# Expert tiles of an attention, MLP and router kernel: three pairs of tiles first, weights standing and 256 rows moving

## What is computed

```python
def _attn_ref(q, k, v):            # q, k, v: 4 x 8 x 768 x 64
    for t in range(S):
        state = gamma * state + outer(k[:, :, t], v[:, :, t])
        y[:, :, t] = scale * (q[:, :, t] @ state)
def _moe_ref(x, w_in, w_out, alpha):       # x: 3072 x 512, w_in: 512 x 2048
    h = x @ w_in
    return (max(h, 0) + alpha * min(h, 0)) @ w_out
def _moe2_ref(x, expert_emb, tau, w1, w2): # 8 experts, w1: 512 x 1024, w2: 1024 x 512
    expert_idx = argmax(cosine(x, expert_emb) / tau, axis=1)
    gate_w = softmax(...)[expert_idx]
    for e in range(E):
        mask = expert_idx == e
        out[mask] = gate_w[mask, None] * (relu(x[mask] @ w1[e]) @ w2[e])
```

## Time and profile before

| | us |
|---|---|
| median of 3 runs | 961.7 |
| lowest, highest | 961.6, 962.18 |
| the profiled execution | 962.25 |
| its span, first to last instruction | 959.8 |
| TensorE busy in the span | 948.4 |
| VectorE, ScalarE, GpSimd busy | 578.9, 255.4, 242.5 |

### The profile page before, as it was taken

The page is one execution under the profiler, slowest core; times in us unless marked ns, Lnnn a source line. Parts: engine busy times, 40 slices in busy tenths (PEclk is TensorE's granted clock), DMA queues, the critical chain, the costliest instruction groups (busy, mean ns, idle before and its releaser), DMA issues.

```text
span 959.8 us, 16536 instructions
## 1 busy us (share of the span) xinstructions
PE 948.4 (99%) x5444; PEld 792.3 (83%) x5445; DVE 578.9 (60%) x1078; ACT 255.4 (27%) x404; POOL 242.5 (25%) x192
## 2 busy tenths in 40 slices
PE   8999999999999999999999999999999999999996
PEld 7888888888888888888888888888888888888885
DVE  5556579647973698469865878674332742523541
ACT  4222121112111211112111212332334543423541
POOL 4443214341433133413432223320000100000001
PEclk9999999999999999999999999999999999999998
DMA  8431296023001400140002203437331471423411
GB/s 306 158 132 56 89 393 223 1 88 132 0 0 57 162 0 0 44 153 1 1 27 74 110 22 132 154 118 267 132 133 44 145 279 44 145 102 117 139 42 54
DMA packets 27121, 102.58 MB, mean 107 GB/s; under 512 B 4383, under 2 KB 4767, under 8 KB 22448
## 3 DMA queue, kind: packets, MB, share of 16 engines
q1 hardware_dynamic: 19280, 83.01, 24.4%
q0 software_dynamic: 4336, 12.61, 3.4%
q10 hardware_dynamic: 3456, 6.32, 2.2%
HBM read 89.30 MB, written 26.30 MB: 120 GB/s over the span
## 4 chain that ended last, share of the span: by engine, by line
PE 94%; issue 3%; DMA 1%; POOL 0%; DVE 0%; SPq 0%; POOLq 0%; ACT 0%
PE bank L694 28%; PE bank L712 27%; PE bank L822 15%; PE bank L787 14%; PE bank L589 2%; PE bank L802 2%; PE bank L633 2%; PE bank L605 2%; PE bank L679 1%; PE bank L622 1%; DMA attention<-in_qk 1%; DMA expert_rows<-rows,slot_i 0%; POOL expert_rows L1553 0%; DVE en_all L908 0%; DMA rows<-expert_rows 0%
## 5 line engine op out<-in xcount | busy, mean ns | idle before, releaser
L694 PE MATMUL bank<-activations_split,weights_split 128*128 128x512 f32 x1152 | 277.9, 391 | 0.0
L712 PE MATMUL bank<-weights_split,activations_split 128*128 128x512 f32 x1152 | 276.3, 389 | 0.0
L712 PEld LDWEIGHTS bank<-weights_split,activations_split 128*128 128x128 f32 x1152 | 216.1, 188 | 45.1 <-POOL activations_split L1535 0.4
L694 PEld LDWEIGHTS bank<-activations_split,weights_split 128*128 128x128 f32 x1152 | 215.0, 188 | 45.8 <-issue 1.1
L1535 POOL TENSOR_TENSOR activations_split<-scratch,activations_split 128x512 fp32r<-128x512 f32 x84 | 116.9, 1391 | 313.1 <-ACT activations_split L1314 302.5
L1314 ACT CAST activations_split<-scratch 128x512 fp32r<-128x512 f32 x96 | 59.8, 623 | 412.2 <-DVE scratch L951 412.2
L822 PE MATMUL bank<-weights_split,activations_split 128*128 (+1 forms) x648 | 160.6, 397 | 0.0
L787 PE MATMUL bank<-weights_split,activations_split 128*128 (+1 forms) x648 | 153.2, 390 | 0.0
L787 PEld LDWEIGHTS bank<-weights_split,activations_split 128*128 128x128 f32 x648 | 121.1, 188 | 24.7
L822 PEld LDWEIGHTS bank<-weights_split,activations_split 128*128 128x128 f32 x648 | 118.0, 188 | 22.5
L1010 DVE SCALAR_TENSOR_TENSOR attention<-rows,en_all 128x512 f32<-128x512 f32 x140 | 135.1, 1007 | 1.0 <-DMA en_all<-en_rows 1.0
(11 more groups left out here) (186 smaller groups left out, 671.8 us busy)
## 6 DMA issues: line engine op xcount, KB each, us to landing
attention<-in_w_exp SPq DMA_DIRECT2D x24, 1024.0 KB, 4.8
attention<-in_kv SPq DMA_DIRECT2D x43, 256.0 KB, 4.4
expert_rows<-in_pad_rows SPq DMA_DIRECT2D x8, 1285.0 KB, 25.0
en_all<-in_w_exp SPq DMA_DIRECT2D x8, 1024.0 KB, 7.2
rows<-in_w_mlp SPq DMA_DIRECT2D x14, 512.0 KB, 3.3
rows<-expert_rows ACTq DMA_DIRECT2D x24, 257.0 KB, 2.7
attention<-in_qk SPq DMA_DIRECT2D x12, 512.0 KB, 5.5
scratch<-in_qk SPq DMA_DIRECT2D x10, 512.0 KB, 3.7
```

Of the source, the lines that this page charges most:

```text
L694: last = mm(H_ps[f % 2][:, :], win(a, kc, f), x[:, kc, :], start=(k == 0), stop=(k == 3 * KC - 1))
L712: last = mm(bank[j][:, :], x[f % 2][:, j * P:(j + 1) * P], wout(a, f), start=(f == 0 and a == 0 and part_ == "hi"), stop=(f == FB - 1 and ...
```

## The change

Three pairs of tiles, 256 rows of one expert each, come before all others: tiles 0 to 5. Pair 0 is what tiles 0 and 1 were. Which experts and rows the pairs 1 and 2 are is worked out by `choose_pairs` on VectorE, from the counts after five chunks; only full pairs of 256 rows that stand in the table by then are taken, of experts in the kernel's order. Each pair has its weights loaded and split as a "run" of its own (0, 1, 2), also if its expert is that of the pair before; the experts' single tiles are the runs 3 to 10.

In a pair `up_two` takes the place of two tiles' `up`. A 128 x 128 piece of w1 stands and 256 rows (both tiles) move; four groups of 24 such matmuls. The units come out with the unit on the partition, as `expert_down` needs them, so a pair has no `h_transpose`; `h_two_high` (ScalarE) and `h_two_low` (VectorE) make the parts straight from PSUM. The table holds the single tiles only (`LEAD` = 6 fewer), each expert's rows in pairs taken off its count; an expert keeps at least one single tile. The splits of runs 1, 2 and 3 stand written out between the pairs' steps. The single tiles' loops start at tile 8 in place of 4. For the five-chunk counts the router's rank step of chunk 4 has one more matmul, and the last scatter to the table waits until pair 1's rows are loaded.

TensorE:

```diff
-                if isinstance(c, int) and c == NC - 3:
+                if isinstance(c, int) and NC - 3 <= c < NC - 1:
...
+                last.then_inc(s_M1, 1)
+            def up_two(i, g, between=None):
+                slot = i % 2 * HALF
+                if g == 0:
+                    pe.wait_ge(s_el, due(s_el, 2 * i + 2))
+                    if i == 0:
+                        pe.wait_ge(s_phi, due(s_phi, 2))
+                        pe.wait_ge(s_plV, due(s_plV, 2))
+                    else:
+                        pe.wait_ge(s_lo[0], due(s_lo[0], HC * i))
+                if i or g >= 2:
+                    pe.wait_ge(s_hl, due(s_hl, 4 * i + g - 1))
+                for j in range(2):
+                    fc, k = 2 * g + j, 0
+                    for kc in range(KC):
+                        for a, b in ((0, 0), (1, 0), (0, 1)):
+                            last = mm(EH_ps[g % 2][:, j * 2 * P:(j + 1) * 2 * P],
+                                      W[:, slot + w1_at(kc, a) + fc * P:slot + w1_at(kc, a) + (fc + 1) * P],
+                                      ex_two[:, b, :, kc * P:(kc + 1) * P], start=(k == 0), stop=(k == 3 * KC - 1))
+                            k += 1
+                        if between is not None and kc % 2 and (j, kc) != (1, KC - 1):
+                            between(2 * j + kc // 2)
                 last.then_inc(s_M1, 1)
                 if between is not None:
-                    between(KC - 1)
+                    between(3)
...
-            pe.wait_ge(s_phi, due(s_phi, 2))
-            pe.wait_ge(s_plV, due(s_plV, 2))
-            up(0, 0, 0, 0)
+            up_two(0, 0)
             for j in range(B):
                 last_transpose(j)
-            up(0, 0, 1, 0, between=last_logits)
-            up(1, 1, 0, 0)
+            up_two(0, 1, between=last_logits)
+            up_two(0, 2)
             router_rank(NC - 1)
             mm(CNT_ps, ones, seen[:, :, B], start=True, stop=True).then_inc(s_cnt, 1)
-            h_transpose(0)
-            up(1, 1, 1, 0)
+            up_two(0, 3)
...
-            expert_down(0, 0, 0, between=lambda: h_transpose(1))
-            expert_down(1, 1, 0, between=lambda: x_transpose(0, 2))
+            expert_down(0, 0, None, between=lambda: x_transpose(0, 2))
+            expert_down(1, 1, None, between=lambda: x_transpose(0, 3))
+            for g in range(4):
+                up_two(1, g)
+            expert_down(2, 2, None, between=lambda: x_transpose(1, 0))
+            expert_down(3, 3, None, between=lambda: x_transpose(1, 1))
+            for g in range(4):
+                up_two(2, g)
+            expert_down(4, 4, None)
+            expert_down(5, 5, None, between=lambda: x_transpose(1, 2))
...
+            e = expert_of(LEAD)
+            up(6, 2, 0, e)
+            x_transpose(1, 3)
+            up(6, 2, 1, e)
+            e_next = expert_of(LEAD + 1)
+            up(7, 3, 0, e_next)
+            h_transpose(6)
+            up(7, 3, 1, e_next)
+            x_transpose(2, 0)
+            expert_down(6, 2, e, between=lambda: h_transpose(7))
```

VectorE (of `choose_pairs`, the linked steps are cut):

```diff
+            def h_two_low(i, g):
+                dve.wait_ge(s_hh, due(s_hh, 4 * i + g + 1))
+                ve.scalar_tensor_tensor(two_part(1, g), EH_ps[g % 2][:, :], 0.0, two_part(0, g).bitcast(f32), ALU.max, ALU.subtract)\
+                  .then_inc(s_hl, 1)
...
+                link(ve.tensor_reduce(ntile[o, :], full, AX, ALU.add))
+                link(ve.tensor_tensor_scan(t_end[o, :], ones[o, 0:E], ntile[o, :], 0.0, ALU.mult, ALU.add))
+                link(ve.scalar_tensor_tensor(t_off[o, :], ntile[o, :], -2.0 * P, cap_step[o, :], ALU.mult, ALU.add))
...
+                ve.tensor_scalar(tab[o, T_PEXP:T_PEXP + PAIRS], nx[o, 0:PAIRS], perm[o, 0:1], None, ALU.add).then_inc(s_pair, 1)
...
+            x_lo_part(1, 1)
             rows_out(NC - 1)
-            x_lo_part(1, 1)
+            link, n = chain(s_tc, 13)
+            choose_pairs()
...
             router_norm(NC - 1)
+            h_two_low(0, 0)
             router_choose(NC - 1, LG_ps)
+            h_two_low(0, 1)
             router_gate(NC - 1)
-            relu_half(0)
             router_place(NC - 1)
...
+            h_two_low(0, 2)
+            h_two_low(0, 3)
+            split_expert(1, (0,))
+            x_lo_part(2, 2)
+            split_expert(1, (1, 2))
+            x_lo_part(3, 3)
+            split_expert(1, (3,))
+            h_two_low(1, 0)
...
+            link(ve.tensor_scalar(t_off[o, :], t_end[o, :], float(PAIRS), None, ALU.min))
+            link(ve.tensor_copy(in_pairs[o, 0:1], t_off[o, 0:1]))
+            link(ve.tensor_tensor(in_pairs[o, 1:E], t_off[o, 1:E], t_off[o, 0:E - 1], ALU.subtract))
+            link(ve.tensor_tensor(cnt_step[o, 0:E - 1], in_pairs[o, 1:E], in_pairs[o, 0:E - 1], ALU.subtract))
+            link(ve.scalar_tensor_tensor(cap_step[o, 0:E - 1], cnt_step[o, 0:E - 1], 2.0 * P, cap_step[o, 0:E - 1], ALU.mult, ALU.add))
+            link(ve.scalar_tensor_tensor(row_first[o, :], in_pairs[o, 0:1], 2.0 * P, row_first[o, :], ALU.mult, ALU.add))
...
+            h_two_low(1, 1)
+            by_place(cnt)
...
+            link(ve.scalar_tensor_tensor(ntile[o, :], in_pairs[o, :], -2.0, ntile[o, :], ALU.mult, ALU.add))
...
-            h_lo_part(0, 0)
-            relu_half(1)
+            h_two_low(1, 2)
...
+            h_two_low(1, 3)
...
-            h_lo_part(1, 1)
-            split_expert(1, (0,))
-            x_lo_part(2, 2)
-            split_expert(1, (1,))
-            w1_part(next_expert(2))
-            x_lo_part(3, 3)
-            split_expert(1, (2,))
-            relu_half(2)
-            split_expert(1, (3,))
-            h_lo_part(2, 2)
+            split_expert(2, (0,))
+            x_lo_part(4, 4)
+            split_expert(2, (1, 2))
+            x_lo_part(5, 5)
+            split_expert(2, (3,))
+            for g in range(4):
+                h_two_low(2, g)
+                split_expert(PAIRS, (g,))
+            w1_part(next_expert(LEAD))
+            x_lo_part(6, 2)
+            x_lo_part(7, 3)
+            relu_half(6)
+            h_lo_part(6, 2)
```

SyncE and ScalarE:

```diff
+            sp.wait_ge(s_pair, due(s_pair, 1))
...
+            for n in range(2):
+                r = sp.value_load(tab[0:1, T_PROW + 1:T_PROW + 2], min_val=0, max_val=PAD - 2 * P)
+                sp.dma_start(x_second[n], table[bass.ds(r + n * P, P), 0:DM]).then_inc(s_xld[2 + n], 16)
+                sp.dma_start(tail_second[:, 2 * n:2 * n + 2], table[bass.ds(r + n * P, P), DM:ROW]).then_inc(s_tail2, 16)
+            e = sp.value_load(tab[0:1, T_PEXP + 1:T_PEXP + 2], min_val=0, max_val=E - 1)
             for m in range(NCH):
                 sp.wait_ge(s_phi, due(s_phi, m + 1))
                 sp.wait_ge(s_plV, due(s_plV, m + 1))
                 load_raw(e, m)
...
+            def expert_weights(e, run):
+                for m in range(NCH):
+                    sp.wait_ge(s_lo[m // HC], due(s_lo[m // HC], HC * (run - 2) + m % HC + 1))
+                    settle(run)
+                    load_raw(e, m)
+            expert_weights(sp.value_load(tab[0:1, T_PEXP + 2:T_PEXP + 3], min_val=0, max_val=E - 1), 2)
             table_done(sp)
-            load_rows(sp, 0, 2)
-            load_rows(sp, 0, 3)
-            load_rows(sp, 1, 0)
+            for n in range(2):
+                r = sp.value_load(tab[0:1, T_PROW + 2:T_PROW + 3], min_val=0, max_val=PAD - 2 * P)
+                sp.dma_start(xrow[n][:, :], table[bass.ds(r + n * P, P), :]).then_inc(s_xld[n], 16)
             pads(sp)
             sp.wait_ge(s_pad0, due(s_pad0, 16))
             sp.wait_ge(s_pads, due(s_pads, 16 * E))
...
+            expert_weights(sp.value_load(tab[0:1, T_PERM:T_PERM + 1], min_val=0, max_val=E - 1), PAIRS)
+            sp.wait_ge(s_tab, due(s_tab, 1))
+            load_rows(sp, 1, 2)
+            load_rows(sp, 1, 3)
...
+            h_two_high(0, 2)
+            split_expert(1, (0,))
+            h_two_high(0, 3)
+            split_expert(1, (1,))
+            x_hi_part(2, 2)
+            split_expert(1, (2,))
             y_part(0, 0, 0)
-            x_hi_part(2, 2)
+            split_expert(1, (3,))
+            x_hi_part(3, 3)
             y_part(1, 0, 1)
+            for g in range(4):
+                h_two_high(1, g)
+                split_expert(2, (g,))
+            x_hi_part(4, 0)
+            y_part(2, 0, 2)
+            x_hi_part(5, 1)
+            y_part(3, 0, 3)
+            for g in range(4):
+                h_two_high(2, g)
+                split_expert(PAIRS, (g,))
...
+            w1_part(next_expert(LEAD), LEAD - 1)
+            y_part(4, 1, 0)
+            load_rows(act, 2, 0)
+            x_hi_part(6, 2)
+            y_part(5, 1, 1)
+            relu_half(6)
+            x_hi_part(7, 3)
+            h_hi_part(6, 2)
```

(4 more changed lines are left out.)

208 lines of the change are left out of this document (116 added, 92 removed).

## The result

The changed kernel takes 958.41 us (median of 7 runs, 957.85 to 958.92); before it was 961.78 us in the same rounds. The ratio is 0.9964, 95% interval 0.9952 to 0.9976: 3.4 us or 0.35% faster. The predicted time was 957.1 us with a range of 955.2 to 961.0, so the measured one lies inside, 1.3 us above the point.

A forecast was written before the change was run, and what follows sets the result against it. TensorE, 99% busy, was taken as the bound. Terms -5.3 - 0.4 + 0.1 + 0.2 + 0.3 + 0.5 = -4.6 us against the median of 961.7 gave 957.1 us; range 955.2 to 961.0 (some 0.83).

The forecast's parts named there:

- What bounds the kernel: Whole kernel: TensorE, busy 99% of the 959.8 us span; only its own work and newly added waits count.
- The transposes, -5.3 us: Tiles 0 to 5: the unit transposes removed, six times 0.89 us, all on TensorE's path.
- The wait for rows, -0.4: TensorE's 0.43 us wait at 642.44 goes, as the third tile's rows come much earlier.
- The 256-column matmul, 0.114 us, +0.1 us: Pairs' up: 288 matmuls of 256 columns at 0.114 us replace 144 of 512; 0.110 gives -1.0, 0.120 gives +1.9.
- The overlap rule: Skill's rule against the change: loads overlap only across row groups, so 214 ns a matmul, up-stage some 29 us longer.
- The count matmul, +0.2: Chunk 4's router: one count matmul added on TensorE, +0.22 us.
- The first low part, +0.3 us of stall: Run-in, about 625 us: choose_pairs delays VectorE's low step to 625.8; TensorE's third group, reached at 625.5, stalls 0.3 us.
- The third run, +0.5 us: Third pair, from about 667 us: VectorE has 0.3 us spare, then 2.97 against TensorE's 2.74 a group; stall 0.5 us (0 to 2.5).
- A chunk of weights in 4.8 us: Weight DMAs: a 1 MB chunk lands in 4.8 us, 7.2 or more for the last of four together.
- The gain is eaten: Rival: 0.120 us a matmul plus 1 to 2.5 us more VectorE stalls; 959.8 to 963, say 960.5 us; chance 0.16.
- The load does not hide: Rival: weight loads exposed in the pairs' 288 up matmuls, +26 us (983) or +31 us (988); chance 0.07.
- The extra tile: Rival: an expert with all rows in pairs keeps a padding tile, 12.25 us more, 969 us; chance 0.02.

The follow-up runs named there:

- e1: The changed kernel with eight 128x128 transposes put back into each of the pairs' six downs: 963.46 us, ratio to before 1.002.
- e9: The changed kernel plus nine groups of 48 matmuls behind its last tile, standing width varied: 256 moving took 0.120 us with 128 standing, 0.113 with 32.
- e6: The changed kernel plus nine groups of 48 matmuls behind its last tile, widths varied: 0.228 us each at 512 moving, 0.120 at 256, 0.111 at 128.
- e3: The changed kernel with five more linked small steps on VectorE at the head of choose_pairs: 960.14 us.
- e2: The changed kernel with rows standing and 512 columns of w1 moving in the pairs' up, units of tiles 0 to 5 wrongly oriented: 957.76 us.
- e10: The changed kernel itself, unedited, run again: 958.64 us, ratio to before 0.9972.
- e4: The changed kernel with ten more linked small steps on VectorE at the end of the tile table: 959.37 us.

## Why the prediction held, and where it was off

**What bounds the kernel:** right. TensorE stays at 99%, and what counted was its own work.

**The transposes, -5.3 us:** right. e1 gives 5.29 against the profile without the gap, 5.06 against the one with it.

**The wait for rows, -0.4:** right, it is gone, and it was worth more than its row said: the 24 matmuls down ahead of it took 6.13 us until the next group (636.31 to 642.44), and the same 24 take 5.56 now (635.26 to 640.82). That is 0.6 us.

**The 256-column matmul, 0.114 us, +0.1 us:** this term was mis-sized. It is 0.120, so 288 x 0.120 = 34.6 against 32.7, +1.9 us: the ceiling that the prediction gave, and 1.8 us above its term, more than the 1.3 us between forecast and result. The value was picked near the warm-up's rate and half of 0.227; but the warm-up's float32 records are another kind of matmul, and (0.50 - 0.27) / 2 is 0.115 and not 0.11, so this row did not bear out the 0.110 of its lower bound. The logits' row had already shown a load of 0.11 us, as long as the stream, and with the two as long as each other 0.120 was measured, 0.0065 over the stream alone. The prediction's ceiling came from a fixed cost per matmul; e9 shows that the number was right and the reason was not. The sign that it gave for being right, groups of 24 that start 2.7 to 2.8 us apart, was missed with 2.88.

**The overlap rule:** the Trainium skill, TensorE: Matmul & The Clock Gate, section "The mechanism" (not the section that the prediction names), says that loads overlap running matmuls only where the row group differs. The trace disagrees: all loads here use all rows, and 0.120 us for 256 columns is 0.10 short of load plus stream (0.22). Of the load 0.0065 us shows. By the formula of the Trainium skill, TensorE: Matmul & The Clock Gate, section "LDWEIGHTS (loading the stationary operand)", 128 columns would take 107 ns (an estimate from that page); the floor in e6 is 0.111 us a matmul.

**The count matmul, +0.2:** as said; the five-chunk counts cost two more records of 0.11 us, in chunk 4's router, ahead of the run-in.

**The first low part, +0.3 us of stall:** did not come. VectorE's timeline of the changed kernel there, answering to the earlier trace rows:

```profile
624.75 0.69 DVE L1248 SCALAR_TENSOR_TENSOR activations_split<-bank,activations_split 128x512 fp32r<-128x512 f32 x1
625.83 0.19 DVE L1091 TENSOR_TENSOR L<-bank,inv 128x32 f32<-128x32 f32 x1 [0.40 <-PE bank L690]
```

The low part ended at 625.44, TensorE's third group began at 625.65. Of 4.22 us idle 0.40 are left: the cover was nearly used up, as said, and e3 shows that one more microsecond would have been a wait. TensorE got there 0.15 us later and VectorE 0.4 us earlier than in the prediction's schedule.

**The third run, +0.5 us:** did not come either. The low part of tile 5's rows ended at 666.34 against 667.38, 1.0 us spare and not 0.3, since TensorE was 0.5 later, by its own matmuls, and VectorE 0.3 earlier; a group of 24 at 2.88 us also just holds VectorE's 2.89 (672.87 to 675.76). The slower matmul paid for these stalls beforehand; in e2, with quicker ones, some of them appear.

**A chunk of weights in 4.8 us:** in the pairs it was 7.8 (14 issues; by the page's DMA rows 4.8 before). The schedule had room for most of it; ScalarE waited 1.0 and 0.5 us for chunks at 681 and 684, and so tile 6's low part, behind these splits, came to be what TensorE waited for in e2.

By its own terms with the measured sizes the sum is -5.3 - 0.6 + 1.9 + 0.2 + 0.3 (the gap at 690 in this profile) = -3.5 us. The two profiles give -3.95 + 0.2 (the count matmul, ahead of that stretch) = -3.7, the medians -3.4. So it closes to some 0.3 us and no better: the run-in starts at 614.7 to 615.8 us in the traces of kernels whose work up to there is the same.

That the forecast came within 1.3 us is partly luck. The matmul was 1.8 us too cheap and the gap of 0.3 us was not in it; the 0.8 us of stalls that did not come and 0.2 us of the wait went the other way.

**The rivals:** "The gain is eaten" was half of it: the 0.120 came, the stalls did not, and each excludes the other in part. (By its own terms this rival reaches from 959.9 to 961.4 us, and not to 963.) "The load does not hide" is refuted as a whole by e6 and e9 and true for 0.0065 us of 0.111. The extra tile did not arise: 27 scatters of output stand in the new page too.

## What to carry to other kernels

Count a change of roles in a matmul by both its streams: when the moving side gets as short as the load of the standing side, look up both (here 0.1135 and 0.111 us, and 0.120 for the two together, 6% over the longer), and take them from the same kind of matmul. Before a saving on the bounding engine is booked in full, look at what the helpers need per group: here 2.89 us of VectorE stood behind 2.88 us of TensorE, and a quicker TensorE got only a part of its 1.9 us (0.65 by the times of e2, 0.8 by the pairs in its trace against e10's) until three steps on three engines were moved. Work that makes another engine late is best priced by adding small steps to it and seeing where the first wait shows.

## What the hardware showed unexpectedly

A wait of 0.67 us, right behind a stretch with the router's small matmuls between half groups, cost more than itself: in the profiled execution of e3 the granted clock fell to 1.2 GHz for 3.4 us and came back, and the group behind the wait took 1.5 us more. Six of the ten runs were 1.2 us or more above the other four; only the slowest has a profile. The wait of 0.79 us in e4, behind full-width matmuls mostly, left the clock alone in the profiled execution; three of e4's ten runs took 960.0 us or more and have no profile. Whether the small matmuls ahead make the difference was not tried.
